# Attention ahead of a mixture of experts and an MLP: where the exponent stands in ScalarE's step

## The chip, the cores and the metric

One core of a Trainium2 chip runs the whole program. The metric is the device time of one execution in microseconds (us); of several executions the median counts. The engines of the core work side by side, each through its own list in order, and wait for each other on semaphores: TensorE (PE in the profile; its weight loads are PEld), VectorE (DVE), ScalarE (ACT), GpSimd (POOL) and SyncE (SP), which only issues transfers.

## The reference

Inputs are q, k and v of shape 4 x 8 x 576 x 64 (batch, heads, sequence, head width) and tau = 0.02, and the weights of two later stages.

```
scores = q @ k.T / sqrt(64)
scores = where(scores >= max(scores) - tau, scores, -1e9)
attn   = exp(scores - max(scores));  attn /= sum(attn) + 1e-9
x      = attn @ v                     # 2304 x 512 after merging the heads
x      = gate * (relu(x @ w1[e]) @ w2[e])     # e: the best of 8 experts for each token
out    = (h * sigmoid(1.702 * h)) @ w_out,  h = x @ w_in     # 512 -> 2048 -> 512
```

## The kernel before

The kernel has three stages: attention (to about 360 us of the span), routing and the experts, and the MLP. The change lies in the attention stage only.

**Units of attention.** The 32 heads are taken in 16 pairs. The two sequences of a pair are cut into 9 units of 128 query rows (U = 9): units 0 to 3 of the first head, unit 4 which holds the last 64 rows of both, units 5 to 8 of the second. There are 144 units. Two pairs form a quad of 18 steps; the first quad and the last ones are written out, the quads between are a hardware loop. In step n (u = n mod 9) each engine does its part for several units at once:

- TensorE, `step` at L1183: `transpose` (L1106), then `score` (L1129), then in u = 1 and u = 5 `values` (L1147), and in u = 3 and u = 7 `turn` (L1161). `transpose` turns four blocks of the probabilities of unit n - 5 into the PSUM tile `pt_ps` (L1109 by way of a helper, four of 128x128), then two blocks of q and k for the next pair (L1123), then the fifth block of the probabilities. The first four wait for `keys_copied`: ScalarE has copied out the four blocks of the step before. The q and k blocks wait for `turned_copied`: all of `pt_ps` of the step before is copied. `score` multiplies q by k for unit n into one of two PSUM tiles `s_ps` (four matmuls at L1143, eight in u = 4) and waits until VectorE has read unit n - 2. `values` multiplies the probabilities of half a finished pair by v (20 matmuls at L1157, into `o_ps`).
- VectorE, `step` at L693: L704 reads the scores of unit n, writes them negated and scaled to one of three `scores` slots and leaves the row minimum in `row_low`. In u = 4 and u = 8 it writes an output tile (L673). Then `mask` (L660, instruction L664) multiplies the exponents of unit n - 2 by "score within tau of the maximum" and sums the rows; its result is what TensorE transposes three steps later. In u = 2 it also takes a reciprocal (L717, L720).
- ScalarE, `step` at L952, which the change touches. In u = 2 and u = 6 it copies the attention output from PSUM (L961), which waits for `pv_done`, the end of `values` one step earlier. Then `copy_turned` (L934) empties `pt_ps`: L938 copies the four blocks after `keys_turned`, L941 the fifth and L949 the q and k blocks (L945 to L947 in u = 4) after `turned`. Last in the step stands the exponent of unit n - 1 (L975), which waits for `low_ready`: VectorE has the minimum of unit n - 1. Its second wait, on `turned`, asks for the transposes of the step before.
- GpSimd, `step` at L581: it adds tau to each row minimum (L589), and four times a pair it splits q and k into parts (L539, L541, u = 2 and 5) or swaps halves of k (L549, L551, u = 1 and 6).

The order on each engine is written out by hand as above; nothing is planned at run time. `pt_ps` has one copy, `s_ps` two, `scores` three and `probs` six.

Of the kernel before, what the change touches and what calls it, by code (L numbers as in the profile page):

```python
# [7 lines left out]
ACT = mybir.ActivationFunctionType  # L8
# [11 lines left out]
def attention_moe_mlp_kernel(nc, q, k, v, tau, modality_id, w_gate, modality_bias, w1, w2, w_in, w_out, out):  # L20
    BATCH, HEADS, SEQ, DH = q.shape
# [9 lines left out]
    U = 2 * TPB - 1  # L31
# [4 lines left out]
    UNITS = PAIRS * U  # L36
    STEPS = 2 * U
    LAG = 5
    SCORE_SLOTS = 3
    PROB_SLOTS = 6  # L40
# [28 lines left out]
    with ctx:  # L69
        def sb(name, shape, dt=F32):  # L70
            return ctx.enter_context(nc.sbuf_tensor(name, shape, dt))
# [4 lines left out]
        def sem(name):  # L76
            return ctx.enter_context(nc.semaphore(name))
# [7 lines left out]
        def put(name, shape, dt=F32, at=None):  # L85

            if at is not None:
                placed[0] = at
            size = 1
            for n in shape[1:]:  # L90
                size *= n
            t = nc.alloc_sbuf_tensor_at(name, shape, dt, offset=slab_at + 4 * placed[0])
            placed[0] += -(-size // 8) * 8
            assert placed[0] <= SLAB, (name, placed[0])
            return t
# [3 lines left out]
        scores = put("scores", [P, SCORE_SLOTS, SEQ])  # L99
# [5 lines left out]
        probs = put("probs", [P, PROB_SLOTS, SPAD])  # L105
# [100 lines left out]
        row_low = sb("row_low", [P, 2, U])  # L206
# [32 lines left out]
        low_ready = sem("low_ready")  # L239
        thresh_ready = sem("thresh_ready")  # L240
        exp_ready = sem("exp_ready")
# [4 lines left out]
        turned = sem("turned")  # L246
# [74 lines left out]
        def wait(eng, s, value):  # L321

            if not isinstance(value, int) or value > 0:
                eng.wait_ge(s, value)

        def on(value, low, high):

            return not isinstance(value, int) or low <= value < high
# [603 lines left out]
        def _(act):  # L932

            def copy_turned(m, v, tj, tu, with_probs, with_qk):  # L934

                if with_probs:
                    act.wait_ge(keys_turned, m - U - LAG + 1)
                    act.copy(pT[:, 0:TAIL, v * P:(v + 1) * P], pt_ps[:, 0:TAIL]).then_inc(keys_copied, 1)  # L938
                act.wait_ge(turned, m + 1)
                if with_probs:  # L940
                    ins = act.copy(pT[:, TAIL, v * P:(v + 1) * P], pt_ps[:, TAIL])  # L941
                if with_qk:
                    at = slice(tu * P, (tu + 1) * P)
                    if tu == TAIL:
                        act.copy(qkT[tj][:, 0, TAIL * P:TAIL * P + LAST], pt_ps[:, QK_AT, 0:LAST])  # L945
                        act.copy(qkT[tj][:, 0, U * P + LAST:(U + 1) * P], pt_ps[:, QK_AT, LAST:P])
                        ins = act.copy(qkT[tj][:, 1, at], pt_ps[:, QK_AT + 1])  # L947
                    else:
                        ins = act.copy(qkT[tj][:, :, at], pt_ps[:, QK_AT:QK_AT + 2])  # L949
                ins.then_inc(turned_copied, 1)  # L950

            def step(quad):  # L952
                for i in range(STEPS):
                    n = quad * STEPS + i
                    j, u = i // U, i % U
                    pair = quad * 2 + j
                    if u in (2, 6) and on(pair, 1, PAIRS + 1):
                        side = 0 if u == 2 else 1
                        wait(act, pv_done, pair * 2 - 1 + side)
                        wait(act, o_written, pair * 2 - 2)  # L960
                        act.copy(oT[:, side * UP:(side + 1) * UP], o_ps[:, 0:UP]).then_inc(oT_copied, 1)  # L961
                    if on(n, LAG, UNITS + LAG) or on(n, 0, UNITS - U):
                        if u == LAG and on(n, LAG, UNITS + LAG):
                            wait(act, pv_done, pair * 2 - 1)
                        if u == 0 and on(n, LAG, UNITS + LAG):
                            wait(act, pv_done, pair * 2 - 2)
                        if u == 0 and on(n, 0, UNITS - U):
                            wait(act, scores_ready, n)
                        copy_turned(n + U, (u - LAG) % U, 1 - j, u, on(n, LAG, UNITS + LAG), on(n, 0, UNITS - U))
                    if on(n, 1, UNITS + 1):  # L970
                        k = (i - 1) % STEPS
                        wait(act, low_ready, n)

                        wait(act, turned, n + U - 1)
                        act.activation(probs[:, k % PROB_SLOTS, 0:SEQ], scores[:, k % SCORE_SLOTS], ACT.Exp,  # L975
                                       bias=row_low[:, k // U, k % U:k % U + 1], scale=-1.0).then_inc(exp_ready, 1)

            for m in range(U):
                copy_turned(m, 0, 0, m, False, True)
# [1 line left out]
            act.dma_start(y_dram[(SLOTS - 1) * P:SLOTS * P], zeros[:]).then_inc(slot_y_stored, 16)  # L981
            act.wait_ge(tau_ready, 5)
            over_quads(act, step, QUADS + 1)

            act.wait_ge(shifted_ready, 1)
# [372 lines left out]
```

## Time and profile before

| | |
|---|---|
| runs of the kernel before | 1086.19, 1085.1, 1088.7 us; median 1086.19 |
| profiled execution | 1090.26 us, its span 1088.5 us |
| TensorE over the span | 990.1 us busy (91%) |
| VectorE, ScalarE, GpSimd | 491.9 (45%), 451.3 (41%), 227.1 us (21%) |
| exponents, L975 | 144 of 796 ns, 30.2 to 346.1 us |
| masks, L664, and minima, L704 | 144 of 954 ns, 144 of 818 ns |

Shares over the whole span mix three stages with different limits. The attention stage is read from the windows and the timelines of its steady part. In a timeline a row gives the start in us, the duration, the engine, the line, the operation with what it writes and reads, and in brackets how long the engine had been idle and what ended that.

### The profile page before, as it was taken

Reading aid. Unit: us, or ns where it says so; the run is one execution under the profiler, and the core shown is the slowest. Engines: PE = TensorE matmul, PEld = TensorE weight load, DVE = VectorE, ACT = ScalarE, POOL = GpSimd, SP = SyncE. Lnnn points to the kernel's source line nnn. Section 1 sums busy time; section 2 is a strip of 40 time slices with the busy share of each in tenths; the row PEclk is TensorE's granted clock in tenths of the full one; section 3 lists DMA queues with packets and bytes.
Section 4 is the critical chain, followed back from the end, with each engine's and each line's share of the span. In section 5 each row is a group of like instructions: output and inputs, shape, how many; then the busy total and the mean of one; then the engine's idle time right before and its main releaser. Section 6 shows DMA issues by size and latency. Waiting matters only on the chain.

```text
span 1088.5 us, 18245 instructions
## 1 busy us (share of the span) xinstructions
PE 990.1 (91%) x5702; PEld 837.3 (77%) x5703; DVE 491.9 (45%) x1065; ACT 451.3 (41%) x1022; POOL 227.1 (21%) x353
## 2 busy tenths in 40 slices
PE   2899999999998359999998685999999999999997
PEld 0777877877886248888887564998999999989996
DVE  1778878878887542212221414543223232232221
ACT  1778877877876032222221423442222222222212
POOL 3655555555552000100010002010010100100000
PEclk9999999999999669999999896999999999999999
DMA  3122222222240072111111323211001010010101
GB/s 71 41 55 58 65 53 61 61 55 62 70 163 23 23 267 98 44 43 48 39 39 39 134 84 110 68 59 30 1 30 28 29 29 0 29 29 0 30 1 29
DMA packets 99968, 59.72 MB, mean 55 GB/s; under 512 B 83680, under 2 KB 83680, under 8 KB 99936
## 3 DMA queue, kind: packets, MB, share of 16 engines
q1 hardware_dynamic: 94016, 44.11, 15.4%
q0 software_dynamic: 3040, 9.96, 2.9%
q10 hardware_dynamic: 2880, 5.24, 1.3%
q8 instruction: 17, 0.28, 0.1%
q14 instruction: 15, 0.12, 0.0%
HBM read 40.95 MB, written 18.35 MB: 54 GB/s over the span
## 4 chain that ended last, share of the span: by engine, by line
PE 81%; DVE 5%; issue 4%; POOL 4%; DMA 2%; ACT 2%; SPq 1%; DVEq 0%; ACTq 0%; POOLq 0%
PE s_ps L1312 19%; PE s_ps L1295 12%; PE s_ps L1229 10%; PE o_ps L1248 10%; PE o_ps L1157 7%; PE o_ps L1295 6%; PE pt_ps L1109 6%; PE s_ps L1143 6%; PE pt_ps L1123 2%; DVE probs L664 2%; PE s_ps L1237 1%; POOL qk_parts L541 1%; PE pt_ps L1281 1%; PE pt_ps L1219 1%; POOL k_swap L551 1%
## 5 line engine op out<-in xcount | busy, mean ns | idle before, releaser
L913 DVE TENSOR_TENSOR g<-s_ps,sig 128x384 f32<-128x384 f32 x96 | 53.5, 558 | 277.2 <-ACT sig L1081 277.2
L1081 ACT ACTIVATE sig<-s_ps 128x384 f32<-128x384 f32 x96 | 47.2, 492 | 285.1 <-PE s_ps L1312 285.1
L704 DVE TENSOR_SCALAR_CACHE_REDUCE scores<-s_ps,taus 128x576 f32<-128x576 f32 x144 | 117.8, 818 | 73.9 <-PE s_ps L1143 50.7
L664 DVE SCALAR_TENSOR_TENSOR probs<-scores,thresh,probs 128x576 f32<-128x576 f32 x144 | 137.2, 954 | 0.0
L1312 PE MATMUL s_ps<-yT_high,w_in_high 128*128 (+1 forms) x384 | 132.4, 345 | 1.4 <-DVE yT_low L887 1.2
L1109 PE MATMUL pt_ps<-ident,probs 128*128 128x128 f32 x720 | 126.9, 277 | 4.7 <-ACT pT L938 2.7
L1312 PE MATMUL s_ps<-yT_high,w_in_low 128*128 (+1 forms) x384 | 130.4, 340 | 0.0
L1312 PE MATMUL s_ps<-yT_low,w_in_high 128*128 (+1 forms) x384 | 129.8, 338 | 0.0
L975 ACT ACTIVATE probs<-scores,row_low 128x576 f32<-128x576 f32 x144 | 114.7, 796 | 17.1 <-DVE scores L704 16.1
L1109 PEld LDWEIGHTS pt_ps<-ident,probs 128*128 128x128 f32 x720 | 83.6, 140 | 28.3 <-issue 21.3
L1143 PE MATMUL s_ps<-qkT 128*128 128x288 f32 x320 | 102.3, 337 | 2.3 <-POOL k_swap L551 2.3
L589 POOL TENSOR_TENSOR thresh<-row_low,taus 128x1 f32<-128x1 f32 x144 | 73.2, 509 | 136.9 <-DVE scores L704 128.2
L1157 PE MATMUL o_ps<-pT,vv 128*64 128x320 f32 x640 | 93.2, 437 | 0.8 <-ACT pT L938 0.8
L1143 PE MATMUL s_ps<-k_swap,qkT 128*128 128x288 f32 x320 | 89.7, 296 | 0.0
L938 ACT COPY pT<-pt_ps 128x512 f32<-128x512 f32 x144 | 84.8, 589 | 8.5 <-PE pt_ps L1109 5.4
L1123 PE MATMUL pt_ps<-ident,qk_parts 128*128 128x128 f32 x288 | 59.3, 290 | 22.3 <-DMA turn_and_gate<-in_moe_w_gate_dram 9.3
L1229 PE MATMUL s_ps<-w_high,slot_xT_high 128*128 128x512 f32 x152 | 63.2, 416 | 17.0 <-DVE w_low L841 17.0
L1312 PEld LDWEIGHTS s_ps<-yT_high,w_in_high 128*128 128x128 f32 x384 | 73.0, 190 | 5.5 <-DVE yT_low L887 1.6
L1295 PE MATMUL s_ps<-w_out_high,g_low 128*128 128x512 f32 x192 | 76.2, 397 | 0.0
L1295 PE MATMUL s_ps<-w_out_low,g_high 128*128 128x512 f32 x192 | 75.8, 395 | 0.0
L1312 PEld LDWEIGHTS s_ps<-yT_low,w_in_high 128*128 128x128 f32 x384 | 73.0, 190 | 3.1
L1295 PE MATMUL s_ps<-w_out_high,g_high 128*128 128x512 f32 x192 | 74.7, 389 | 0.3 <-DVE g_low L895 0.3
(165 smaller groups left out, 1842.7 us busy)
## 6 DMA issues: line engine op xcount, KB each, us to landing
w_raw<-in_moe_w_dram SPq DMA_DIRECT2D x16, 512.0 KB, 4.8
y_dram<-slot_y ACTq DMA_DIRECT2D x19, 256.0 KB, 2.0
x_dram<-xs SPq DMA_DIRECT2D x16, 288.0 KB, 2.7
out_dram<-out_sb SPq DMA_DIRECT2D x36, 128.0 KB, 2.4
qk<-in_q_dram SPq DMA_DIRECT2D x32, 128.0 KB, 2.2
qk<-in_k_dram SPq DMA_DIRECT2D x32, 128.0 KB, 2.5
w_in_raw<-in_moe_w_in_dram SPq DMA_DIRECT2D x4, 1024.0 KB, 5.0
w_out_raw<-in_moe_w_out_dram SPq DMA_DIRECT2D x16, 256.0 KB, 2.6
```

The source lines that it names most:

```text
L664: dve.scalar_tensor_tensor(out=probs[:, i % PROB_SLOTS, 0:SEQ], in0=scores[:, i % SCORE_SLOTS], scalar=thresh[:, j, u:u + 1], in1=probs[:, ...
L704: dve.tensor_scalar(scores[:, i % SCORE_SLOTS].rearrange("p (c n) -> p c n", c=2), s_ps[i % 2][:, :, 0:HALF], taus[:, 3:4], None, ALU.mult ...
L938: act.copy(pT[:, 0:TAIL, v * P:(v + 1) * P], pt_ps[:, 0:TAIL]).then_inc(keys_copied, 1)
L975: act.activation(probs[:, k % PROB_SLOTS, 0:SEQ], scores[:, k % SCORE_SLOTS], ACT.Exp, bias=row_low[:, k // U, k % U:k % U + 1], scale=-1. ...
L1109: return pe.transpose(pt_ps[:, block], probs[:, k % PROB_SLOTS, block * P:(block + 1) * P], ident[:])
L1123: mm = pe.transpose(pt_ps[:, QK_AT + c], qk_parts[:, tu, c].rearrange("p a d -> p (a d)").bitcast(F32), ident[:])
L1143: mm = pe.matmul(s_ps[i % 2][:, c, 0:HALF], qkT[j][:, 0, q_tile * P:(q_tile + 1) * P], keys[:, first:first + HALF], start=(at == 0), stop= ...
L1157: mm = pe.matmul(o_ps[lo:lo + DH, 0:UP], vv[j][:, side, block], pT[:, block, at:at + UP], start=(block == 0), stop=(block == TPB - 1))
L1229: mm = pe.matmul(slot_h_ps[:, c], x_part[:, a, :], w_part[:, a, cols], start=(a == 0 and part == 0), stop=(a == DB - 1 and part == 2))
L1248: mm = pe.matmul(o_ps[:], h_part[:, f, :], w_part[:, f], start=(f == 0 and part == 0), stop=(f == FB1 - 1 and part == 2))
L1295: mm = pe.matmul(mlp_y_ps[i], g_part[:, f % GT, at], w_part[:, f, :], start=(f == 0 and part == 0), stop=(f == FB2 - 1 and part == 2))
L1312: mm = pe.matmul(mlp_h_ps[f % 2], w_part[:, a, f * P:(f + 1) * P], y_part[:, bass.ds(c % 2 * DB + a, 1)].rearrange("p a b -> p (a b)"), st ...
```

## The change

In ScalarE's step the exponent moves from the end to the front: it now precedes the copy of the attention output and the copies of the transposes of the same step. Its operands, its waits and the semaphore it raises stay as they are.

```diff
                     pair = quad * 2 + j
+                    if on(n, 1, UNITS + 1):
+                        k = (i - 1) % STEPS
+                        wait(act, low_ready, n)
+
+                        wait(act, turned, n + U - 1)
+                        act.activation(probs[:, k % PROB_SLOTS, 0:SEQ], scores[:, k % SCORE_SLOTS], ACT.Exp,
+                                       bias=row_low[:, k // U, k % U:k % U + 1], scale=-1.0).then_inc(exp_ready, 1)
                     if u in (2, 6) and on(pair, 1, PAIRS + 1):
...
                         copy_turned(n + U, (u - LAG) % U, 1 - j, u, on(n, LAG, UNITS + LAG), on(n, 0, UNITS - U))
-                    if on(n, 1, UNITS + 1):
-                        k = (i - 1) % STEPS
-                        wait(act, low_ready, n)
-
-                        wait(act, turned, n + U - 1)
-                        act.activation(probs[:, k % PROB_SLOTS, 0:SEQ], scores[:, k % SCORE_SLOTS], ACT.Exp,
-                                       bias=row_low[:, k // U, k % U:k % U + 1], scale=-1.0).then_inc(exp_ready, 1)
```

## Rows read from the trace of the kernel before

**Rows 1.** The page: TensorE's busy time, and its granted clock in 40 slices.

```profile
PE 990.1 (91%) x5702; PEld 837.3 (77%) x5703; DVE 491.9 (45%) x1065; ACT 451.3 (41%) x1022; POOL 227.1 (21%) x353
...
PEclk9999999999999669999999896999999999999999
```

**Rows 2.** Windows: busy time by engine, clock, DMA; start-up and a steady stretch.

```profile
core 0: us, PE busy (x) PEld busy (x) DVE busy (x) ACT busy (x) POOL busy (x), PEclk, DMA share, GB/s
...
34.00:46.00 12.00, 8.97 (x68) 7.63 (x66) 11.21 (x23) 8.70 (x22) 8.57 (x12) 1.00 0.22 49
...
160.00:200.00 40.00, 39.58 (x306) 31.62 (x304) 32.66 (x79) 31.76 (x81) 22.23 (x35) 1.00 0.26 59
```

**Rows 3.** Waits from 40 to 320 us: total us, times, longest.

```profile
PE s_ps L1143 <- POOL k_swap L551: 2.3, 7, 0.5
...
ACT oT L961 <- PE o_ps L1157: 36.9, 27, 1.9
ACT probs L975 <- DVE scores L704: 12.8, 28, 1.3
```

**Rows 4.** Timeline of TensorE from 194 to 242 us.

```profile
199.81 0.66 PE L1109 MATMUL pt_ps<-ident,probs 128*128 128x128 f32 x4
...
206.23 0.63 PE L1109 MATMUL pt_ps<-ident,probs 128*128 128x128 f32 x4
206.69 0.38 PE L1123 MATMUL pt_ps<-ident,qk_parts 128*128 128x128 f32 x2
...
207.64 2.91 PE L1157 MATMUL o_ps<-pT,vv 128*64 128x320 f32 x20
210.49 0.66 PE L1109 MATMUL pt_ps<-ident,probs 128*128 128x128 f32 x4
...
219.89 0.66 PE L1109 MATMUL pt_ps<-ident,probs 128*128 128x128 f32 x4
...
230.85 0.66 PE L1109 MATMUL pt_ps<-ident,probs 128*128 128x128 f32 x4
...
240.14 0.66 PE L1109 MATMUL pt_ps<-ident,probs 128*128 128x128 f32 x4
```

**Rows 5.** Timeline of ScalarE from 194 to 242 us.

```profile
199.92 0.43 ACT L961 COPY oT<-o_ps 128x320 f32<-128x320 f32 x1 [1.71 <-PE o_ps L1157]
...
205.49 0.60 ACT L938 COPY pT<-pt_ps 128x512 f32<-128x512 f32 x1
...
206.11 0.41 ACT L949 CAST qkT<-pt_ps 128x256 fp32r<-128x256 f32 x1
206.79 0.78 ACT L975 ACTIVATE probs<-scores,row_low 128x576 f32<-128x576 f32 x1 [0.27 <-DVE scores L704]
207.47 0.57 ACT L938 COPY pT<-pt_ps 128x512 f32<-128x512 f32 x1
...
214.36 0.59 ACT L938 COPY pT<-pt_ps 128x512 f32<-128x512 f32 x1
...
215.21 0.31 ACT L947 CAST qkT<-pt_ps 128x128 fp32r<-128x128 f32 x1
```

**Rows 6.** Timeline of VectorE from 194 to 242 us.

```profile
204.38 1.30 DVE L664 SCALAR_TENSOR_TENSOR probs<-scores,thresh,probs 128x576 f32<-128x576 f32 x1
...
205.93 0.82 DVE L704 TENSOR_SCALAR_CACHE_REDUCE scores<-s_ps,taus 128x576 f32<-128x576 f32 x1 [0.24 <-POOL thresh L589]
...
208.18 0.82 DVE L704 TENSOR_SCALAR_CACHE_REDUCE scores<-s_ps,taus 128x576 f32<-128x576 f32 x1 [0.24 <-DVE probs L664]
...
208.92 0.82 DVE L664 SCALAR_TENSOR_TENSOR probs<-scores,thresh,probs 128x576 f32<-128x576 f32 x1
...
209.99 0.82 DVE L704 TENSOR_SCALAR_CACHE_REDUCE scores<-s_ps,taus 128x576 f32<-128x576 f32 x1 [0.24 <-ACT probs L975]
...
232.51 0.82 DVE L704 TENSOR_SCALAR_CACHE_REDUCE scores<-s_ps,taus 128x576 f32<-128x576 f32 x1 [1.35 <-PE s_ps L1143]
...
234.61 0.82 DVE L704 TENSOR_SCALAR_CACHE_REDUCE scores<-s_ps,taus 128x576 f32<-128x576 f32 x1
```

## The prediction

> **What bounds the kernel now.** I read the windows first, because the whole-span shares mix three stages: TensorE's 91% and its clock row [rows 1] say that it carries the kernel, not where this change bites. In a steady 40 us of attention TensorE is busy 39.58 us at the full clock of 2.4 GHz, VectorE 32.66, ScalarE 31.76 [rows 2]. So TensorE sets the pace; freeing another engine can give back only TensorE's small gaps, while any new wait in front of TensorE costs in full.
>
> The waits come next. ScalarE idles 36.9 us in 27 waits for the attention output and 12.8 us in 28 waits of the exponent for VectorE's minimum [rows 3]. TensorE has next to no wait on record [rows 3]; it is fed just in time. The second number matters more than it looks: the exponent already arrives at ScalarE before its minimum is there, and today nothing urgent stands behind it.
>
> The timelines give the links. I write T for the start of a step's transposes on TensorE, M for the start of its minimum on VectorE, E for an exponent and C for the first copy of a step on ScalarE.
> - C to next T: 205.49 to 206.23, **0.74 us** [rows 4, 5]. TensorE has no second `pt_ps`, so each copy releases the next transposes.
> - M to E: 205.93 to 206.79, **0.86** [rows 5, 6].
> - E to a copy queued behind it: 206.79 to 207.47, **0.68** [rows 5].
> - T to the same unit's M, if VectorE is free: 230.85 to 232.51, **1.66** after a block of value matmuls [rows 4, 6]; its q and k transposes start up to 0.03 sooner in the other steps, so 1.63 there.
> - M to the next M, VectorE working without a break: 208.18 to 209.99, **1.81**; 232.51 to 234.61, **2.10**, where the reciprocal lies between [rows 6].
>
> **The loop that the change closes.** Nothing is added or removed: 144 exponents, the same copies, the same waits, no transfer. Only the order on ScalarE moves, and with it what queues behind the exponent's wait. Before, the exponent of unit n-1 was last in step n: if its minimum was late, the copies of step n were already out and TensorE had been released. In rows: copy at 205.49, next transposes at 206.23, and the exponent, which had to wait for its minimum, only at 206.79 [rows 4, 5]. After, the copies of step n stand behind that exponent, so
> T(n+1) >= C(n) + 0.74 >= E(n-1) + 0.68 + 0.74 >= M(n-1) + 0.86 + 1.42 = M(n-1) + **2.28**,
> and M(n-1) >= T(n-1) + 1.63. Two steps take at least 3.91 us, 1.96 each. Before, the copies of step n stood only behind the exponent of unit n-2: the same 3.91 us was spread over three steps, 1.30 each, just about TensorE's own step. From 206.23 on, a step without values takes 1.41 to the start of the values (207.64) [rows 4]. That is the whole mechanism: one step of slack is gone.
>
> The values blocks interrupt it. TensorE is busy with 20 matmuls for 2.85 us (207.64 to 210.49) [rows 4]; there ScalarE and VectorE catch up. So I work the sum between them, calling the transposes after the values of u = 5 T6 and after those of u = 1 T2.
>
> *T6 to T2.* M6 = T6 + 1.66. T8 = M6 + 2.28 = T6 + 3.94. M8 = T8 + 1.63 = T6 + 5.57 (VectorE alone would allow 2 x 1.81 after M6, 5.28, so it isn't later). T1 = M8 + 2.28 = T6 + 7.85. From T1 to T2 nothing changes: 206.23 to 210.49, 4.26, for the copies of step 1 are long done when the values end. Sum **12.11**. Before: 199.81 to 210.49 = 10.68 and 219.89 to 230.85 = 10.96, mean 10.82 [rows 4]. **+1.29.**
>
> *T2 to T6.* M2 = T2 + 1.66, M3 = M2 + 2.10 = T2 + 3.76. The copies of step 4 stand behind exponent 3: C4 = M3 + 0.86 + 0.68 = T2 + 5.30. The q and k transposes of step 5 need all of them: from C4 to the end of its last copy 214.36 to 215.52, 1.16 [rows 5], then 0.17 as from 206.52 (206.11 + 0.41) to 206.69 [rows 4, 5]: T2 + 6.63. From those transposes to the end of the values 206.69 to 210.49, 3.80 [rows 4]. Sum 10.43; before 9.40 and 9.29 (210.49 to 219.89, 230.85 to 240.14), so +1.08. A mask beside GpSimd's work takes longer: 204.38 to the next minimum at 205.93 is 1.55, against 1.07 from 208.92 to 209.99 [rows 6], so 0.48. The split of q and k begins at the minimum of u = 2 and overlaps the mask ahead of M3, so part of that 0.48 falls on this path; I take an eighth of a microsecond, +**1.20** in all.
>
> The Trainium skill, "SBUF — State Buffer" (section "SBUF: two separate sides"), holds that a VectorE operation with two SBUF inputs and a GpSimd operation that reads SBUF exclude each other for the whole instruction. By that rule the mask ahead of M3 would be held in full, and each T2 to T6 would take the whole 0.48 and not 0.12: 15 x 0.36 = 5 us more.
>
> *Moves with one answer.* The exponent now in front of the output copy (u = 2 and 6) costs nothing: M1 lies 1.63 after T1 and T2 4.26 after it, so the exponent starts 1.8 us ahead of the values' end and is over by then; after u = 5 it is alike. In the rows ScalarE stood idle 1.71 us there [rows 5]. If that cover went, it would be 0.68 on that step. The exponent's wait on `turned` concerns a step whose copies are done. Masks get their exponents no later relative to the minimum, since the exponent follows the minimum at once; GpSimd's thresholds follow VectorE. SyncE's loads are hidden as before, and later still.
>
> **Sum.** Values come in pairs 1 to 16. There are 15 stretches from T2 to T6 and 15 from T6 to the next T2 (the last of them to the last step with an exponent). 15 x (1.29 + 1.20) = 37.4 us. The first pair has no values; there VectorE is already busy 11.21 of 12.00 us [rows 2] and sets the pace, so the loop adds little: one to three microseconds over nine steps, I take 2. Total **+39.4**. Against the profiled execution's 1090.3 us that is 1129.7 us; against the median of the runs, 1086.2 us, which lies 4.1 us lower, **1126 us**. Routing, experts and MLP only start later.
>
> **The rivals.**
> *A, a gain.* Today each exponent after a copy delays the next copy by 0.68; after the values ScalarE has to catch up and TensorE waits for it (206.23 comes 0.74 after the copy at 205.49: TensorE was held). With the exponent done during the values this could vanish. Worth at most what TensorE has as gaps, 0.3 to 0.4 us a half quad, 16 of them: 5 to 6 us, **1080 us**. For it: the 36.9 us idle. Against it: the loop above, which needs only that the minimum comes 1.66 after its transposes, and every row has it so or later.
> *B, no change.* The exponent waits for VectorE in 28 of 125 steps anyway [rows 3] and ScalarE has a fifth of its time free; if that freedom were in the right place, **1086 us**. It is not: it lies beside the values.
> *C, much slower.* TensorE stretches, masks and GpSimd's operations fall together once more on M3 and on M8: 0.48 more in each stretch, 30 x 0.48 = 14 us, **1141 us**. Decides when both minima, not one, are preceded by a mask of 1.3 us.
> *D, the clock.* TensorE now pauses about 0.5 us in most steps. In the start-up stretch it was busy 8.97 of 12 us and kept 1.00 [rows 2]; the slices at 0.6 and 0.8 [rows 1] lie outside attention. If it fell to 1.2 GHz throughout attention, its 39.58 busy us of 40 would nearly double: up to 300 us over some 310 us of attention, **about 1400 us**. No row here shows a fall in attention.
> The Trainium skill, "TensorE: Matmul & The Clock Gate" (section "A second HAM failure mode: psum-queue depth-cycling"), tells of a kernel in which frequent small pauses between groups of matmuls made the clock go back and forth; that is D in part.
> *E, a small loss.* VectorE's backlog goes away when TensorE slows, and each link comes out at its shortest; half the loss, **1106 us**.
>
> **How the numbers follow.** The forecast with its bounds (E's edge to C) has 0.83; below it with a smaller loss 0.04, C and beyond 0.04 more, D 0.01; A 0.04, B 0.04. Range: low end, a loss of 1.6 us a half quad, 16 x 1.6 = 26, 1112 us, less a little for B's side: 1110. High end: C, 1141. A measurement of this kernel tells about 0.3%, 3 us, from no change. Faster 0.04, same 0.04, slower 0.92.
>
> **What would show it.** In the changed profile: two steps between values take 3.9 us; each C follows its E by 0.68 and each such E its M by 0.86; T6 to T2 near 12.1 and T2 to T6 near 10.5; TensorE waits for L938 where it had none; TensorE's busy share in a steady window falls to about 36 of 40; the wait of the output copy stays near 1 us or more; the clock stays 1.00; times behind attention are unchanged. I am wrong if the next transposes start sooner than 2.2 us after the minimum of two units before, or if a half quad stays near 20.1 us (219.89 less 199.81 [rows 4]).

## The result, and the profile of the changed kernel

| | before | changed |
|---|---|---|
| median of the runs | 1087.06 us (1085.1 to 1088.7, 4 runs) | 1124.74 us (1123.95 to 1126.48, 4 runs) |
| profiled execution, span | 1090.26, 1088.5 us | 1125.17, 1123.3 us |
| start of the last values block | 353.98 us | 391.54 us |

The changed kernel takes **1.035** times as long (95% interval 1.0327 to 1.0373), 37.7 us more. The forecast was 1126 us, its range 1110 to 1141.

The page of the changed kernel, its parts 1 and 2 (busy time; TensorE's granted clock in 40 slices), to be read beside [rows 1]:

```profile
PE 1001.2 (89%) x5702; PEld 837.9 (75%) x5703; DVE 484.6 (43%) x1065; ACT 456.4 (41%) x1022; POOL 228.1 (20%) x353
...
PEclk9999999999999957999999897899999999999999
```

The same instructions and a longer span. TensorE's busy time grew by 11 us with the same 5702 matmuls (the page doesn't say why); the rest of the 34.8 us that the span grew is time in which TensorE stood idle. The window says in which stage (columns as in [rows 2]):

```profile
160.00:200.00 40.00, 36.71 (x273) 27.81 (x272) 27.38 (x70) 28.78 (x72) 19.83 (x29) 1.00 0.22 51
```

TensorE is down from 39.58 to 36.71 of 40 us, and every other engine does less in the same time as well. No engine's share rises, so none has become the bottleneck by its own work. The clock stayed at 1.00, 2.4 GHz.

Who waits for whom (total us, times, longest). First two rows of the kernel before, from 40 to 320 us, to be read beside [rows 3]:

```profile
PE pt_ps L1109 <- ACT pT L938: 0.2, 1, 0.2
...
DVE scores L704 <- PE s_ps L1143: 27.2, 28, 1.4
```

Then the changed kernel, from 40 to 355 us:

```profile
PE pt_ps L1109 <- ACT pT L938: 25.9, 56, 1.5
...
ACT probs L962 <- DVE scores L704: 57.2, 104, 1.3
ACT oT L968 <- PE o_ps L1157: 22.0, 27, 1.1
...
DVE scores L704 <- PE s_ps L1143: 71.9, 49, 2.7
```

TensorE now waits for ScalarE's copy (25.9 us, where it had 0.2), ScalarE's exponent for VectorE's minimum (57.2 us, it was 12.8 in a window only little shorter), VectorE for TensorE's scores (71.9 us, it was 27.2). The three rows name each other in a ring. The output copy's wait shrank from 36.9 to 22.0 us: the exponent did move into that idle time, and nothing was won by it.

The ring with its times, one turn from T2. TensorE, ScalarE and VectorE of the changed kernel, 190 to 240 us:

```profile
210.04 0.66 PE L1109 MATMUL pt_ps<-ident,probs 128*128 128x128 f32 x4
...
213.95 0.63 PE L1109 MATMUL pt_ps<-ident,probs 128*128 128x128 f32 x4 [0.52 <-ACT pT L938]
...
216.61 0.41 PE L1123 MATMUL pt_ps<-ident,qk_parts 128*128 128x128 f32 x2
...
220.44 0.66 PE L1109 MATMUL pt_ps<-ident,probs 128*128 128x128 f32 x4
```

```profile
212.56 0.78 ACT L962 ACTIVATE probs<-scores,row_low 128x576 f32<-128x576 f32 x1 [0.80 <-DVE scores L704]
213.24 0.57 ACT L938 COPY pT<-pt_ps 128x512 f32<-128x512 f32 x1
...
214.65 0.78 ACT L962 ACTIVATE probs<-scores,row_low 128x576 f32<-128x576 f32 x1 [0.40 <-DVE scores L704]
215.33 0.57 ACT L938 COPY pT<-pt_ps 128x512 f32<-128x512 f32 x1
```

```profile
211.70 0.82 DVE L704 TENSOR_SCALAR_CACHE_REDUCE scores<-s_ps,taus 128x576 f32<-128x576 f32 x1 [2.65 <-PE s_ps L1143]
...
213.79 0.82 DVE L704 TENSOR_SCALAR_CACHE_REDUCE scores<-s_ps,taus 128x576 f32<-128x576 f32 x1
```

T2 at 210.04, its minimum at 211.70 (+1.66), the exponent at 212.56 (+0.86), the copy of step 3 at 213.24 (+0.68), T4 at 213.95 (+0.71). Then M3 at 213.79 (+2.09), its exponent at 214.65 (+0.86), the copy of step 4 at 215.33 (+0.68), the q and k transposes of step 5 at 216.61, T6 at 220.44: 10.40 us from T2, where [rows 4] have 9.40 and 9.29. T4 itself is not on this path: M3 follows M2 through VectorE's own work, and it is exponent 3, ahead of the copies of step 4, that holds step 5.

### The profile page after: what moved, and what is told of

Read it like the earlier page. It is cut to its first block, busy times and chain, and to the rows that moved or that the text cites. A ratio compares the mean times of both kernels' runs of the same rounds, so it can differ in the third digit from the quotient of the medians.

```text
span 1123.3 us, 18251 instructions
## 1 busy us (share of the span) xinstructions
PE 1001.2 (89%) x5702; PEld 837.9 (75%) x5703; DVE 484.6 (43%) x1065; ACT 456.4 (41%) x1022; POOL 228.1 (20%) x353
## 4 chain that ended last, share of the span: by engine, by line
PE 80%; issue 7%; DVE 4%; ACT 4%; DMA 1%; POOL 1%; ACTq 1%; SPq 1%; DVEq 0%; POOLq 0%
PE s_ps L1312 18%; PE s_ps L1295 12%; PE s_ps L1229 10%; PE o_ps L1248 9%; PE o_ps L1157 8%; PE o_ps L1295 6%; PE pt_ps L1109 6%; PE s_ps L1143 5%; ACT pT L938 2%; PE pt_ps L1123 2%; PE s_ps L1237 1%; DVE scores L704 1%; DVE probs L664 1%; ACT probs L962 1%; PE pt_ps L1281 1%
## 5 line engine op out<-in xcount | busy, mean ns | idle before, releaser
L1109 PE MATMUL pt_ps<-ident,probs 128*128 128x128 f32 x720 | 129.3, 281 | 31.8 <-ACT pT L938 30.2
L962 ACT ACTIVATE probs<-scores,row_low 128x576 f32<-128x576 f32 x144 | 111.8, 777 | 71.1 <-DVE scores L704 69.1
L1109 PEld LDWEIGHTS pt_ps<-ident,probs 128*128 128x128 f32 x720 | 81.0, 141 | 66.7 <-DVE probs L664 36.3
L664 DVE SCALAR_TENSOR_TENSOR probs<-scores,thresh,probs 128x576 f32<-128x576 f32 x144 | 129.9, 903 | 0.0
L938 ACT COPY pT<-pt_ps 128x512 f32<-128x512 f32 x144 | 82.3, 571 | 6.6 <-PE pt_ps L1109 5.4
```

Source lines behind the costliest of these rows:

```text
L664: dve.scalar_tensor_tensor(out=probs[:, i % PROB_SLOTS, 0:SEQ], in0=scores[:, i % SCORE_SLOTS], scalar=thresh[:, j, u:u + 1], in1=probs[:, ...
L1109: return pe.transpose(pt_ps[:, block], probs[:, k % PROB_SLOTS, block * P:(block + 1) * P], ident[:])
```

## The experiments

All figures are medians in us. The kernel before ran beside each group: 1089.41 in the first, 1087.47 in the second, 1086.92 in the third. "Values to values" is read from the starts of the value matmuls (x20) in TensorE's timeline: T2 to T6 and T6 to T2 are as long as the distance between two such starts. In the kernel before, T2 to T6 takes 9.29 and about 9.42 us in turn and T6 to T2 10.68 and 10.96. The length of attention alone is read from the start of the first routing instruction (L744), 359.0 us in the kernel before and 396.6 in the changed one; each such reading is of one profiled execution.

**1. Which steps carry the loss.** An exponent at the front is allowed in some steps only; `exponent()` is the block that the change moved.

```diff
+                    first = u in (0, 3, 4, 7, 8)
+                    if first and on(n, 1, UNITS + 1):
+                        exponent()
                     if u in (2, 6) and on(pair, 1, PAIRS + 1):
...
                         copy_turned(n + U, (u - LAG) % U, 1 - j, u, on(n, LAG, UNITS + LAG), on(n, 0, UNITS - U))
+                    if not first and on(n, 1, UNITS + 1):
+                        exponent()
```

> The exponent stands first only in the steps u = 0, 3, 4, 7 and 8 and last in u = 1, 2, 5 and 6. Loop theory (a copy of a step behind the exponent of the unit before holds TensorE's next transposes; costs only where no value matmuls follow): these five steps carry the whole loss, about 1125 us, 1120 to 1129. Rival 'every wait counts' (the loss is the sum of ScalarE's waits for the minimum over all nine steps): five ninths of 37.7 us, about 1108 us. Rival 'the output copy' (the loss comes from the exponent ahead of the copy of the attention output): near 1087 us.

Measured: **1124.52**, ratio 1.0331 (1.0314 to 1.0349). The counterpart has `first = u in (1, 2, 5, 6)`:

> The exponent stands first only in the steps u = 1, 2, 5 and 6, the ones beside the value matmuls. Loop theory: the copies of steps 1 and 5 are needed only after 2.85 us of value matmuls, so there it is free; in steps 2 and 6 it costs at most what the minimum of the unit before comes too late for the values' end, 0 to 0.7 us each: 1087 to 1100 us, most likely 1091. Rival 'every wait counts': four ninths of 37.7 us, about 1104 us. Rival 'the output copy': about 1125 us. Rival 'a gain' (the exponent done during the values frees ScalarE afterwards): 1081 us.

Measured: **1091.38**, ratio 1.002 (1.0008 to 1.0032). The five steps without value matmuls behind them carry nearly the whole loss (35.1 us over their base), the four others 2.0 us. In the trace of these four, every other T2 to T6 takes 9.84 us where the kernel before has 9.42; steps 1 and 5 alone (run 6) don't show that, and no run holds step 2 alone. In that second kernel the exponent's waits from 40 to 345 us are these:

```profile
ACT probs L961 <- DVE scores L704: 43.3, 55, 1.5
```

43.3 us of waiting and 2 us of loss; in the kernel with the five steps the same row is smaller and the loss is nearly whole:

```profile
ACT probs L961 <- DVE scores L704: 14.6, 34, 1.3
```

So the total of a wait says nothing of its price. What stands behind the waiting instruction, and when that is needed, does. The rival "every wait counts" falls.

**2. The output copy.** The exponent stands behind the copy of the attention output and ahead of the copies of the transposes.

```diff
                         act.copy(oT[:, side * UP:(side + 1) * UP], o_ps[:, 0:UP]).then_inc(oT_copied, 1)
+                    if on(n, 1, UNITS + 1):
+                        k = (i - 1) % STEPS
+                        wait(act, low_ready, n)
...
                     if on(n, LAG, UNITS + LAG) or on(n, 0, UNITS - U):
```

> The exponent stands behind the copy of the attention output but ahead of the copies of the transposes, in every step. Loop theory: the loop through the copies is closed as in the changed kernel, and in u = 2 and 6 the exponent no longer runs during the values but 0.5 us later than the output copy, so the first transposes after it are held 0.5 us more, which the wait for the minimum two steps on mostly absorbs: 1125 to 1132 us. Rival 'the output copy': most of the loss goes, near 1090 us.

Measured: **1126.11**, ratio 1.0341 (1.0324 to 1.0359). Where all exponents stand ahead of the copies of the transposes, the order against the output copy makes no difference that these runs can tell (1.0341 against 1.035); the order against the copies of the transposes makes the loss.

**3. The two terms apart.** The forecast had priced the two stretches by the exponents ahead of the copies of steps 7 and 0 (T6 to T2) and of step 4 (T2 to T6). Each was left alone in front: `first = u in (7, 0)` and `first = u in (4,)`.

> The exponent stands first only in the steps u = 7 and u = 0. Loop theory with its terms: only the stretch from T6 to T2 is lengthened, 15 times 1.29 us, so 19 us over the kernel before (1087 to 1089 us): 1107 us, 1103 to 1112; T2 to T6 stays near 9.35 us. If instead the cost is shared evenly by the steps where the exponent waits: two ninths of 37.7 us, 1096 us.

> The exponent stands first only in the step u = 4. Loop theory with its terms: only the stretch from T2 to T6 is lengthened, 15 times 1.2 us, 18 us over the kernel before: 1106 us, 1101 to 1110; T6 to T2 stays near 10.8 us or gets up to 0.3 shorter, since VectorE's backlog is gone. Even shares: one ninth of 37.7 us, 1092 us.

Measured: **1110.94**, 23.5 us over its base (ratio 1.0223, 1.0193 to 1.0252), and **1104.16**, 16.7 us over it (1.0155, 1.0128 to 1.0183). Together 40.2 us against the whole change's 37.7; in attention alone 22.6 and 13.9 us, together 36.4 against 37.6. Three of nine exponents hold the loss, to within what the totals can tell. Starts of the value matmuls in TensorE's timeline, u = 5, u = 1 and u = 5 again; first the kernel with steps 7 and 0:

```profile
208.62 2.91 PE L1162 MATMUL o_ps<-pT,vv 128*64 128x320 f32 x20
...
221.23 2.91 PE L1162 MATMUL o_ps<-pT,vv 128*64 128x320 f32 x20
...
230.52 2.91 PE L1162 MATMUL o_ps<-pT,vv 128*64 128x320 f32 x20
```

then the kernel with step 4:

```profile
203.75 2.91 PE L1162 MATMUL o_ps<-pT,vv 128*64 128x320 f32 x20
...
214.43 2.91 PE L1162 MATMUL o_ps<-pT,vv 128*64 128x320 f32 x20
...
224.89 2.91 PE L1162 MATMUL o_ps<-pT,vv 128*64 128x320 f32 x20
```

With steps 7 and 0 the stretch T6 to T2 is 12.61 us (12.07 the next time), on average 0.2 us longer than in the changed kernel, and T2 to T6 is 9.29 every time. With step 4, T2 to T6 is 10.46 (10.39 the next time) and T6 to T2 10.68 every time. Each edit lengthens its own stretch only. The other stretch loses only its longer turns: T2 to T6 no longer takes 9.42 nor T6 to T2 10.96 (the second the forecast of this run had named as possible).

**4. Is VectorE's minimum on the path?** The addition and the reciprocal that lie between M2 and M3 go one step later, in the changed kernel and in the kernel before.

```diff
-                    if u == 2 and on(pair, 1, PAIRS + 1):
+                    if u == 3 and on(pair, 1, PAIRS + 1):
                         wait(dve, probs_ready, pair * U)
```

> The changed kernel with VectorE's reciprocal and its addition (L717, L720) one step later, u = 3 instead of u = 2, so that they no longer lie between the minima M2 and M3. Loop theory: M3 comes 2.10 - 1.81 = 0.29 us sooner and is on the path, 15 times: 4.4 us less than the changed kernel, 1120 us; the same edit in the kernel before gives nothing. If VectorE's minimum is not on the path: no change, 1125 us.

> The kernel before with the same edit on VectorE. Loop theory: the path of the kernel before does not run through M3, 0 to 1 us less: 1086 to 1089 us beside its own base. If VectorE sets the pace in both kernels: 4 us less.

Measured: **1121.28** (ratio 1.0313, 1.0285 to 1.0341, against 1.035 for the changed kernel) and **1089.59** (ratio 1.0018, 1.0 to 1.0035). The two ratios of the first pair overlap, so the totals alone would not decide. The trace does: in the changed kernel with this edit T2 to T6 is 10.11 us (starts at 205.30 and 215.41), 0.29 less than 10.40, and T6 to T2 keeps 12.38 (227.79). 0.29 us was the forecast. In the kernel before the edit gained nothing: 1089.59 lies 2.1 us above its base, where 0 to 1 us less was forecast, and in the trace T6 to T2 went from 10.68 and 10.96 to about 10.86 and 11.25. So the 0.29 us ahead of M3 is not on the path of the kernel before, but the two instructions are not free at their later place; I did not follow which wait they lengthen there. In the changed kernel they have their full price ahead of M3.

**5. Between the copies.** The exponent comes after the copy of the four blocks, which releases TensorE's next four transposes, and ahead of the copies of the fifth block and of q and k.

```diff
                     act.copy(pT[:, 0:TAIL, v * P:(v + 1) * P], pt_ps[:, 0:TAIL]).then_inc(keys_copied, 1)
+                if between is not None:
+                    between()
                 act.wait_ge(turned, m + 1)
```

> The exponent stands between the copy of the four blocks and the copies of the fifth block and of q and k. Loop theory: TensorE's four transposes are released early, but its q and k transposes wait for the copies behind the exponent: minimum + 0.86 + 0.68 + 0.55 + 0.17 = 2.26 us to the q and k transposes, 1.8 us to the step's start, where the changed kernel has 2.28; T6 to T2 about 11.15, T2 to T6 about 9.95, so about 14 us over the kernel before: 1101 us, 1095 to 1110. Rival 'only the four-block copy closes the loop': near 1087 us. Rival 'any place ahead of the last copy costs the same': near 1125 us.

Measured: **1119.54**, ratio 1.0283 (1.0264 to 1.0302), outside my range. Its ScalarE, from T2 at 205.94 on:

```profile
206.64 0.59 ACT L938 COPY pT<-pt_ps 128x512 f32<-128x512 f32 x1 [0.15 <-PE pt_ps L1114]
207.12 0.78 ACT L963 ACTIVATE probs<-scores,row_low 128x576 f32<-128x576 f32 x1
207.80 0.26 ACT L943 COPY pT<-pt_ps 128x128 f32<-128x128 f32 x1
207.94 0.38 ACT L951 CAST qkT<-pt_ps 128x256 fp32r<-128x256 f32 x1
```

and TensorE's next q and k transposes:

```profile
208.38 0.44 PE L1128 MATMUL pt_ps<-ident,qk_parts 128*128 128x128 f32 x2 [0.38 <-ACT qkT L951]
```

The exponent starts the moment the first copy lets it, with no wait in brackets: its minimum was long there. TensorE waits all the same, for the cast that ended at 208.32. I had counted only the loop through VectorE. There is a second path, on ScalarE alone: transposes, first copy, exponent, last copy, next q and k transposes, 205.94 to 208.38 = 2.44 us, of which the exponent is 0.68; those are followed 0.92 us later (209.30) by whatever TensorE has next. Two such steps take 3.36 us, where two of 1.41 [rows 4] take 2.82. To tell the two apart, each step held the exponent of unit n-2 in the same place, whose minimum is a whole step older:

```diff
-                        k = (i - 1) % STEPS
-                        wait(act, low_ready, n)
-                        wait(act, turned, n + U - 1)
+                        k = (i - 2) % STEPS
+                        wait(act, low_ready, n - 1)
+                        wait(act, turned, n + U - 2)
```

> As the run with the exponent between the copies, but each step holds there the exponent of unit n-2, whose minimum is long known. New theory for the miss of that run: ScalarE's own time closes a second loop, from a step's transposes through the first copy, the exponent (0.68 us) and the last copy to the next q and k transposes, whether or not the minimum is late: the loss stays, 1110 to 1120 us, most likely 1117. If the wait for the minimum made the loss, it goes: 1087 to 1093 us.

Measured: **1117.63**, ratio 1.0281 (1.0258 to 1.0303). ScalarE has no wait for the minimum left in its list; the two largest of 40 to 345 us are

```profile
ACT oT L970 <- PE o_ps L1162: 61.7, 27, 2.3
ACT pT L938 <- PE pt_ps L1114: 21.3, 50, 1.2
```

and TensorE waits as before (0.38 us at 206.23). T2 to T6 and T6 to T2 take 10.25 and 11.88 us here, 10.26 and 11.89 in the run before it: the late minimum had no part. Here the loss is ScalarE's own time inside the turn of `pt_ps`, not a late input.

**6. Is there a gain in it?** The exponent stands first only in u = 1 and 5, or only in u = 6.

> The exponent stands first only in the steps u = 1 and u = 5, whose copies are needed only after the value matmuls. Loop theory: free and of no use, within 3 us of the kernel before (1086 to 1091 us). Rival 'every wait counts': two ninths of 37.7 us, 1096 us.

> The exponent stands first only in the step u = 6, where ScalarE idled 1.5 to 1.7 us before the output copy in the kernel before; afterwards ScalarE is one exponent ahead in the run of steps 7, 8, 0 and 1, in which TensorE waits 0.3 us for it. Rival 'a gain': 15 times 0.3 us less, 1083 us. Loop theory: minimum 5 comes 0.9 to 1.1 us ahead of T6, so the copies of step 6 come 0.2 to 0.4 us later, about what is won: 1085 to 1091 us.

Measured: **1088.73**, ratio 1.0021 (1.0007 to 1.0035), and **1088.49**, ratio 1.0015 (0.9999 to 1.0031). Neither is faster. The values block of the last step with an exponent starts at 346.81 us in the kernel before, 346.74 and 346.08 in these two, so attention is as long as it was or under a microsecond shorter. Even that microsecond is not a gain of the order: in the second kernel the first values block starts at 45.31 us, 1.4 sooner than before, and from there on it takes 300.77 us, where the kernel before takes 300.13. What the totals add lies outside attention or in the measurement; I can't say which. No version here beats the kernel before.

## Why the prediction was right

**What bounds.** TensorE was the bound, and new waits ahead of it lengthened the kernel, although every other engine had time to spare: right.

**The loop.** M to E 0.86, E to C 0.68, C to T 0.71 in the rows above: 2.25 from a minimum to the second next transposes, forecast 2.28. The run of the five steps and its counterpart show that this order alone makes the loss, and moving M3 by 0.29 us moved T6 by 0.29 us, as this chain has it. What it left out is a second turn on ScalarE alone, which needs no late minimum (run 5); in the changed kernel itself the minimum was the later of the two, by ScalarE's waits for it (0.80 and 0.40 us in the rows above). No run puts an older exponent, of unit n - 2, at the front, so how much of the 37.7 us would stay without the late minimum is open.

**T6 to T2.** Forecast 12.11 us, measured 11.91 (198.13 to 210.04) and 12.40 (220.44 to 232.84), mean 12.16: +1.33 for +1.29. That the mean comes so near is partly luck: one is 0.20 below the sum, the other 0.29 above it. The term that was off is T8 to M8, forecast 1.63: 1.51 in the first (201.94 to 203.45), 1.97 in the second (224.35 to 226.32). Between them lies one long mask, the very term of rival C, which came in every other stretch from T6 to T2:

```profile
224.77 1.30 DVE L664 SCALAR_TENSOR_TENSOR probs<-scores,thresh,probs 128x576 f32<-128x576 f32 x1
...
226.32 0.82 DVE L704 TENSOR_SCALAR_CACHE_REDUCE scores<-s_ps,taus 128x576 f32<-128x576 f32 x1 [0.24 <-POOL thresh L589]
```

**T2 to T6.** Forecast 10.43 and an allowance of 0.12 for masks beside GpSimd's split; measured 10.40, +1.05 for +1.20. The allowance was not needed, and still less the whole 0.48: the split started at 213.25, when the mask ahead of M3 (212.44 to 213.25) was just over. The long mask came one step later, behind M3.

**The start-up.** I took 2 us for the first pair; the first values block starts 3.3 us later (46.68 to 49.99). There the copies of q and k alone already stand behind the exponent. From that block to the one of the last step with an exponent it is 300.13 us before and 334.38 after (49.99 to 384.37): 34.3 us, where 15 x 2.49 = 37.4 stood in the sum. Of these, T6 to T2 has 19.6 us (forecast 19.4) and T2 to T6 14.7 (forecast 18.0). The last stretches, without q and k transposes, gained less than the others. The 3.3 us are uncertain by about 1.3: in run 4's edit of the kernel before, which changes nothing ahead of that block, it starts at 45.38. The two misses cancel in part: the attention stage ends 37.6 us later by its last values block, forecast 39.4.

**After attention.** Forecast unchanged. The first routing instruction (L744) starts at 359.0 and at 396.6 us; the rest takes 729.5 us before and 726.7 after in these two executions. It holds no changed instruction. In the thirteen profiles of this case, whose edits all lie in attention, the rest takes from 725.5 to 731.3 us, so the 2.8 us are within its scatter; they are why the spans of these two executions differ by 34.8 us only.

**The moves costed at nothing.** The exponent ahead of the output copy: free in the changed kernel, by run 2; in the counterpart of run 1 it cost, together with the exponents of steps 1 and 5, 2.0 us. The exponent ahead of the output copy of u = 2 starts at 208.34 and the values end near 210.1, 1.8 us later as worked out. After u = 5 it is not quite alike: 219.15, and the values end near 220.5, 1.35 us later, and the output copy waits 0.63 us there. The sign "near 1 us or more" holds after u = 1 only.

**The rivals.** A and B fell with the first result, and A once more in run 6. C's half microsecond came in six of the thirty stretches, all from T6 to T2; no long mask lay ahead of M3. E fell too: the loss was 37.7 us, not half. D did not happen: with 56 recorded waits of TensorE for the copy, the longest 1.5 us, the granted clock was 1.00 in the windows of attention. By the Trainium skill, "TensorE: Matmul & The Clock Gate" (section "A second HAM failure mode: psum-queue depth-cycling"), small pauses between groups of matmuls made the clock of another kernel go back and forth; this trace shows no such thing, with a TensorE that is still busy 36.71 of 40 us.

## What to carry to other kernels

Before moving a waiting instruction forward in an engine's list, write down what will stand behind its wait and who needs that next. An instruction whose input tends to be late belongs behind the work that releases the busiest engine, even where its engine idles a fifth of the time. And price a wait by the turn that it closes, in steps: the same 3.9 us over three steps was hidden here, over two steps it cost 3.5% of the kernel. Nor is it enough that the input is ready: inside the turn of `pt_ps`, between the copies, an exponent with no wait at all cost 2.8% (run 5), while ahead of the value matmuls a late one cost next to nothing (runs 1 and 6).

## What I had not expected

When VectorE's mask and GpSimd's cast fall together, one of the two is held up, and which one seems to hang on a tenth of a microsecond. In one stretch of the changed kernel the mask at 202.22 took 0.81 us and GpSimd's cast took 1.18; one stretch later the mask took 1.30 (above) and the same cast 0.66:

```profile
202.22 0.81 DVE L664 SCALAR_TENSOR_TENSOR probs<-scores,thresh,probs 128x576 f32<-128x576 f32 x1
...
202.38 1.18 POOL L551 CAST k_swap<-qkT 64x576 fp32r<-64x576 f32 x1 [0.17 <-POOL k_swap L549]
...
224.79 0.66 POOL L551 CAST k_swap<-qkT 64x576 fp32r<-64x576 f32 x1 [0.17 <-POOL k_swap L549]
```

The sum of the two durations is 1.99 and 1.96 us: the overlap costs the same, only its bearer changes, and half a microsecond more or less in every other stretch from T6 to T2 comes with it. It agrees with the Trainium skill, "SBUF — State Buffer" (section "SBUF: two separate sides"), by which one of the two, the one that starts first, holds the shared ports for its whole instruction. The recorded starts alone don't tell which one that is: the mask's is the earlier both times, by 0.16 us where the cast was held and by 0.02 where the mask was. The same two cases, with leads of 0.16 or 0.17 and of 0.01 or 0.02 us, come back in turn from 112 to 340 us. That the lead decides is my reading of these rows; no run changed it.

In the kernel before the price falls on the other bearer. There the long mask (204.38, [rows 6]) lies in the shorter stretch from T6 to T2, 10.68 us, and the long cast in the longer one, 10.96: it took 1.17 us from 224.69 on, and TensorE's scores of u = 0 waited 0.31 us for it. Which of the two had better be held depends on whose result is wanted next.
